# The first attention head's preparation divided anew over the engines, and the low parts of the probabilities dealt out by key tile in another way

## What is computed

```python
def _attn_ref(q, k, v):                      # 2 x 8 heads, 1152 keys, head_dim 64
    q_pool = q.reshape(B, H, S // 2, 2, D).mean(axis=3)      # 576 queries per head
    scores = scale * np.matmul(q_pool, k.transpose(0, 1, 3, 2))
    scores = scores - np.max(scores, axis=-1, keepdims=True)
    attn = np.exp(scores)
    attn = attn / (np.sum(attn, axis=-1, keepdims=True) + 1e-09)
    return np.matmul(attn, v)
def _moe_ref(x, w_in, w_out):                # 1152 tokens, 512 -> 2048 -> 512
    h = x @ w_in
    return (h * np.tanh(softplus(h))) @ w_out
def _moe2_ref(x, w_in, w_out):
    h = x @ w_in
    return np.where(h > 0, h, np.exp(h) - 1) @ w_out
```

## Time and profile before

| | us |
|---|---|
| median of 3 runs | 705.71 |
| lowest and highest | 703.37, 706.11 |
| profiled execution | 703.71 |
| its span | 701.9 |

### The profile page before, as it was taken

One profiled execution on the slowest core, in us unless ns is written; L12 is line 12 of the kernel. 1 busy time (PEld: TensorE's weight loads), 2 busy tenths in 40 slices (PEclk: granted clock), 3 DMA queues, 4 the chain that ended last, 5 costly groups with the idle time before them and its releaser, 6 DMA issues.

```text
span 701.9 us, 12236 instructions
## 1 busy us (share of the span) xinstructions
PE 657.8 (94%) x3984; PEld 636.7 (91%) x3984; DVE 423.4 (60%) x620; ACT 397.0 (57%) x743; POOL 426.5 (61%) x388
## 2 busy tenths in 40 slices
PE   3589999999999999999999999999999999999997
PEld 2478889898898988899999999999999999999997
DVE  6667878787887876377777665777543332223222
ACT  2357888888888878755555555555643322222221
POOL 4266788888888866587786666787644422222221
PEclk9599999999999999999999999999999999999999
DMA  5355564555556540012220000122222110001001
GB/s 162 96 155 157 147 174 135 163 159 158 143 147 163 157 110 16 16 50 71 62 61 0 0 0 30 48 67 67 60 77 61 46 45 0 0 0 46 1 1 45
DMA packets 31503, 54.30 MB, mean 77 GB/s; under 512 B 4752, under 2 KB 10208, under 8 KB 31456
## 3 DMA queue, kind: packets, MB, share of 16 engines
q1 hardware_dynamic: 31296, 53.66, 27.7%
q10 hardware_dynamic: 160, 0.04, 0.0%
HBM read 30.93 MB, written 2.36 MB: 47 GB/s over the span
## 4 chain that ended last, share of the span: by engine, by line
PE 67%; POOL 8%; ACT 8%; DVE 7%; issue 7%; DMA 2%; SPq 1%; POOLq 0%; ACTq 0%; DVEq 0%
PE py L490 9%; PE py L491 8%; PE py L492 8%; PE pH L475 8%; PE pH L476 8%; PE pH L477 8%; PE pm L398 5%; DVE part_max L712 3%; PE po L430 3%; PE po L431 3%; PE po L432 3%; PE ps L413 3%; PE ps L414 3%; POOL pl L931 3%; ACT ph L565 2%
## 5 line engine op out<-in xcount | busy, mean ns | idle before, releaser
L986 POOL TENSOR_TENSOR gl<-fg,gh 128x384 fp32r<-128x384 f32 x96 | 97.3, 1014 | 142.4 <-ACT gh L655 141.1
L931 POOL TENSOR_TENSOR pl<-p,ph 128x576 fp32r<-128x576 f32 x72 | 106.0, 1480 | 67.4 <-ACT p L571 63.3
L712 DVE TENSOR_REDUCE part_max<-pm 128x2 f32<-128x768 f32 (+1 forms) x123 | 111.1, 904 | 39.9 <-PE pm L398 38.1
L490 PE MATMUL py<-gh,wout_h 128*128 128x384 f32 x384 | 129.2, 336 | 3.6 <-DVE xl L842 2.2
L491 PE MATMUL py<-gl,wout_h 128*128 128x384 f32 x384 | 128.4, 334 | 0.0
L492 PE MATMUL py<-gh,wout_l 128*128 128x384 f32 x384 | 128.3, 334 | 0.0
L477 PE MATMUL pH<-xh,win_l 128*128 (+1 forms) x384 | 128.3, 334 | 0.0
L475 PE MATMUL pH<-xh,win_h 128*128 (+1 forms) x384 | 128.3, 334 | 0.0
L476 PE MATMUL pH<-xl,win_h 128*128 (+1 forms) x384 | 128.3, 334 | 0.0
L565 ACT ACTIVATE ph<-ps 128x576 fp32r<-128x576 f32 x144 | 93.9, 652 | 51.2 <-PE ps L414 48.8
L821 DVE RECIPROCAL fi<-fp 128x192 f32<-128x192 f32 x48 | 64.9, 1353 | 52.2 <-POOL fp L994 52.1
(11 more groups left out here) (68 smaller groups left out, 1367.7 us busy)
## 6 DMA issues: line engine op xcount, KB each, us to landing
kh<-k_hi SPq DMA_DIRECT2D x60, 144.0 KB, 2.6
w_raw<-w_in SPq DMA_DIRECT2D x32, 256.0 KB, 2.7
w_raw<-w_out SPq DMA_DIRECT2D x32, 256.0 KB, 2.6
k_pack<-kP SPq DMA_DIRECT2D x16, 288.0 KB, 3.2
q_raw<-qT SPq DMA_DIRECT2D x16, 288.0 KB, 3.1
v_raw<-v SPq DMA_DIRECT2D x16, 288.0 KB, 2.9
kl<-k_pack SPq DMA_DIRECT2D x32, 144.0 KB, 2.4
q<-q SPq DMA_DIRECT2D x16, 144.0 KB, 2.5
```

The costliest lines, as they stand in the source:

```text
L490: pe.matmul(out, hi, gh[:, f % 4, :], start=(f == 0), stop=False)
L712: dve.tensor_reduce(part_max[:, par, 2 * g:2 * g + wide], group_banks(n, g)[:, 0:wide, 0:MC], AX.X, ALU.max).then_inc(m_read, 1)
L931: pool.tensor_tensor(pl[:, ph_slot(slot, kt), :], p32[:, p32_slot(n, kt) % 3, :], ph[:, ph_slot(slot, kt), :].bitcast(F32), ALU.subtract). ...
```

## The change

Start of the program: VectorE sums and rounds head 0's q, and makes both halves of `q1`; keys' upper halves are written by VectorE and the lower ones by ScalarE; the constant row of `kl` is set by ScalarE, the presets of `vt` by GpSimd; SyncE loads q first. Three groups of maxima of head 1 stand ahead of head 0's scores, and ScalarE's preparation of head 2 ahead of the exponentials. Semaphores of presets and of the k loads are doubled, one for each parity.

Steady part: `POOL_KT` gives GpSimd tiles 1, 3, 5, 7 (and 8 in even heads). At tiles 6 and 7 scores and group stand ahead of the value matmuls, as they did at tiles 0 to 5; at tile 8 they still follow. Steps of the division and of the preparation stand at other tiles, and VectorE does the division's steps ahead of `split_p` of the same tile.

```diff
-POOL_KT = ((2, 4, 5, 6, 8), (2, 4, 5, 8))
+POOL_KT = ((1, 3, 5, 7, 8), (1, 3, 5, 7))
-FIRST_GROUPS = (2, 2, 2, 2, 0, 1, 1, 1, 2)
+EARLY_GROUPS = 3
+FIRST_GROUPS = (2, 1, 1, 1, 1, 1, 1, 1, 1)
 GROUPS = (1, 1, 1, 0, 1, 1, 1, 1, 1)
-VECTOR_AT = {"scale": (1, None), "invert_0": (3, None), "invert_1": (5, None), "finalize": (None, 3)}
+VECTOR_AT = {"scale": (0, None), "invert_0": (3, None), "invert_1": (4, None), "finalize": (None, 0)}
...
-GPSIMD_AT = {"split_v": (0, 0), "multiply_sums": (1, None), "sum_q": (3, 3), "split_w": (4, 4),
-             "split_k": (6, 6), "split_q": (7, 7), "split_x": (None, 7)}
+GPSIMD_AT = {"split_v": (1, 1), "multiply_sums": (1, None), "split_w": (3, 3), "sum_q": (3, 3),
+             "split_x": (None, 5), "split_k": (6, 6), "split_q": (8, 8)}
...
                     nxt = ahead(n, kt)
-                    if kt + AHEAD < KT:
+                    if kt == KT - 1:
+                        pv(n, kt)
+                    if nxt is not None:
                         scores(*nxt)
-                        for head, g in groups_at(n, kt):
-                            max_group(head, g)
+                    for head, g in groups_at(n, kt):
+                        max_group(head, g)
+                    if kt < KT - 1:
                         pv(n, kt)
-                    else:
-                        pv(n, kt)
-                        if nxt is not None:
-                            scores(*nxt)
-                        for head, g in groups_at(n, kt):
-                            max_group(head, g)
...
-            preset_scores(0)
+            for par in range(2):
+                dve.memset(kl[par][D:2 * D, :].bitcast(F32), 0.0).then_inc(kl_preset[par], 1)
+                dve.memset(q2[par][D:2 * D, :].bitcast(F32), 0.0).then_inc(q2_preset[par], 1)
+            dve.wait_ge(q_in, 16)
+            dve.tensor_tensor(q_sum[:, :], q_raw[:, 0, :], q_raw[:, 1, :], ALU.add).then_inc(q_summed, 1)
+            dve.wait_ge(q_summed, 1)
+            dve.tensor_copy(q_hi[:, :], q_sum[:, :]).then_inc(first_rounded, 1)
+            dve.wait_ge(first_rounded, 1)
+            for part, cols in ((slice(0, D), slice(0, HQ)), (slice(D, 2 * D), slice(HQ, SQ))):
+                dve.tensor_copy(q1[D:2 * D, 0, cols], q_hi[part, :].bitcast(F32)).then_inc(q1_spread, 16)
+                dve.tensor_tensor(q1[0:D, 0, cols], q_sum[part, :], q_hi[part, :].bitcast(F32),
+                                  ALU.subtract).then_inc(q1_spread, 16)
             dve.wait_ge(k_rounded, 1)
-            for rows in (slice(0, D), slice(D, 2 * D)):
-                for part, cols in ((slice(0, D), slice(0, HK)), (slice(D, 2 * D), slice(HK, SK))):
-                    dve.tensor_copy(kh[0][rows, cols], k_hi[part, :].bitcast(F32)).then_inc(kh_spread, 16)
+            for part, cols in ((slice(0, D), slice(0, HK)), (slice(D, 2 * D), slice(HK, SK))):
+                dve.tensor_copy(kh[0][0:D, cols], k_hi[part, :].bitcast(F32)).then_inc(kh_spread, 16)
```

More of the change, by code:

```diff
@@ L131, in build @@
         w_rd = [sem(f"w_rd{i}") for i in range(2)]
-        preset, preset_kl, preset_pad, preset_vt = sem("preset"), sem("preset_kl"), sem("preset_pad"), sem("preset_vt")
+        preset_pad = sem("preset_pad")
+        q2_preset, kl_preset, vt_preset = [[sem(f"{name}_preset{i}") for i in range(2)] for name in ("q2", "kl", "vt")]
+        first_rounded = sem("first_rounded")
         preset_row, row_reduced, row_spread = sem("preset_row"), sem("row_reduced"), sem("row_spread")
@@ L135, in build @@
         q1_spread, q2_spread = sem("q1_spread"), sem("q2_spread")
-        kl_spread, k_rounded, kp_in = sem("kl_spread"), sem("k_rounded"), sem("kp_in")
+        kl_spread, k_rounded = sem("kl_spread"), sem("k_rounded")
+        kp_in = [sem(f"kp_in{i}") for i in range(2)]
         sum_prod, sum_inv = sem("sum_prod"), sem("sum_inv")
@@ L222, in groups_at @@
             counts = FIRST_GROUPS if n == 0 else GROUPS
[L223 to L227, removed]
+            before = (EARLY_GROUPS if n == 0 else sum(GROUPS[4:])) + sum(counts[:kt])
             for g in range(before, before + counts[kt]):
@@ L337, in next_q @@
                 load_q(m)
+            load_q(0)
             load_kp(0)
-            load_q(0)
             load_kp(1)
@@ L437, in _ @@
                 max_group(0, g)
-            pe.wait_ge(preset, 1)
-            pe.wait_ge(preset_kl, 2)
+            for g in range(EARLY_GROUPS):
+                max_group(1, g)
+            pe.wait_ge(q2_preset[0], 1)
+            pe.wait_ge(kl_preset[0], 2)
             for kt in range(AHEAD):
@@ L538, in split_q, with preset_sign, first_keys @@
                 act.activation(q_hi[:, :], q_sum[:, :], ACT.Copy).then_inc(qh_done, 1)
+            def preset_sign(par):
+                act.wait_ge(kl_preset[par], 1)
+                act.activation(kl[par][D:D + 1, :], kl[par][D:D + 1, :].bitcast(F32), ACT.Copy, bias=-1.0,
+                               scale=0.0).then_inc(kl_preset[par], 1)
+            def first_keys(cols, part):
+                act.wait_ge(k_rounded, 1)
+                act.activation(kh[0][D:2 * D, cols], k_hi[part, :].bitcast(F32), ACT.Copy).then_inc(kh_spread, 16)
             def split_v(n):
@@ L592, in split_x @@
                 act.activation(x_tile(xh, p), x_pair[:, :], ACT.Copy).then_inc(xh_done, 1)
-            split_q(0)
+            preset_sign(0)
             round_k(0)
+            first_keys(slice(0, HK), slice(0, D))
+            first_keys(slice(HK, SK), slice(D, 2 * D))
             split_v(0)
+            round_k(1)
             split_q(1)
-            round_k(1)
+            preset_sign(1)
             spread_row(0)
+            split_q(2)
+            round_k(2)
             for kt in range(AHEAD):
                 exp_tile(0, kt)
-            split_q(2)
-            round_k(2)
             for n in range(HEADS):
@@ L778, in _ @@
                 max_group(0, g)
-            preset_v(0)
-            preset_scores(1)
-            preset_v(1)
+            for g in range(EARLY_GROUPS):
+                max_group(1, g)
             for kt in range(AHEAD):
@@ L790, in _ @@
                         max_group(head, g)
-                    nxt = ahead(n, kt)
-                    if nxt is not None and nxt[1] in VKT[nxt[0] % 2]:
-                        split_p(*nxt)
                     if at("scale"):
@@ L801, in _ @@
                         finalize(n // 2 - 1)
+                    nxt = ahead(n, kt)
+                    if nxt is not None and nxt[1] in VKT[nxt[0] % 2]:
+                        split_p(*nxt)
             scale_by_partner(PAIRS - 1)
@@ L949, in _ @@
             split_k(1)
+            sum_q(2)
+            split_q(2)
             for kt in range(AHEAD):
```

45 lines of the change are left out of this document (17 added, 28 removed).

## The result

The changed kernel takes 708.08 us (median of 12 executions, 705.65 to 709.70), the one before, beside it on the same chip, 703.95 (median of 12). The ratio is 1.005 with an interval of 1.0033 to 1.0066: 0.5% slower, 3.5 us by the ratio and 4.1 by the medians, where the prediction said 8.4. The time lies inside the range of 700 to 720, just under the forecast's own 708.5 to 718. The profiled execution took 706.97, its span is 705.2 for 701.9.

The account below looks back on a forecast made before the run. Attention heads were taken as bound by TensorE's work (14.6 of 16.1 us) plus waits on chains of small operations. Start −6.3 and steady heads +14.7 gave +8.4, hence 712.1 (profiled) or 714.1 (median), forecast 713 us, range 700 to 720.

Parts of the forecast that it names:

- behind tile 2's subtraction: Steady heads: VectorE subtracts tile 2 ahead of reducing tile 0's group, delaying tile 1's group and value matmuls, +0.8 us per head.
- behind the collision: Steady heads, tile 0: scaling or finalizing meets GpSimd's subtraction of tile 3, delaying tile 2's group, +0.6 us per head.
- given back at tile 5 of odd heads: Odd heads: finalizing no longer stands before the reduction of tile 4's group, so tile 5's group waits less, −0.8 us.
- the steady term: Heads 1 to 15 together: odd heads 17.05 for 16.4, even 17.45 for 16.0, +14.7 us, bounds 7 and 19.
- (a): Start: with casts and presets divided anew, the first maximum matmul comes at 9.8 us, 1.9 earlier.
- (b): Start: three groups of head 1 fit into the row of maxima's 3.6 us trip; first scores 22.3, against 24.16.
- (c): Start: the first value matmul still waits for a double group, 30.7 us against 32.5.
- (d): Head 0: seven single groups, 14.6 us of matmuls and about 2 at the low clock; ends at 47.1 against 51.71.
- R1: Rival, faster: steady heads stay at 16.1 us and only the start counts, 699 us; chance 0.17.
- R2: Rival, near no change: wait behind tile 2 but no collision, 0.5 us per head, 707 us; chance 0.15.
- R3: Rival, slower: row of maxima's margin fails, 0.3 us per head more, or start gains 3; 718 us; with R4 0.14.
- R4: Rival: start gets no shorter because q or the GpSimd subtraction comes late, 717 us; chance with R3 0.14.

Follow-up runs that it names:

- e13: Changed kernel, with GpSimd's subtraction of tile 3 waiting, from head 2 on, until VectorE's scaling or finalizing is over: 701.74 us, 0.9963 of the kernel before.
- e6: e4 with the new POOL_KT as the only change in its steady part: 708.78 us, 1.007 of the kernel before.
- e3: Changed kernel with TensorE's old order at tiles 6 and 7, value matmuls ahead of scores and group: 709.13 us, 1.0061 of the kernel before.
- e11: e4 with the loads of the first weights and head 1's v behind the copies of head 2's keys and queries: 693.7 us, 0.9846 of the kernel before.
- e12: e4 with finalizing at the odd head's tile 1, ScalarE's split_x at tile 3, and the loads placed as in e11: 690.27 us, 0.9784 of the kernel before.
- e14: e10 with the loads placed as in e11: 688.84 us, 0.9773 of the kernel before.
- e8: e4 without the three early groups of maxima, head 0 with double groups again: 703.43 us, 0.9999 of the kernel before.
- e10: e4 with finalizing at the odd head's tile 1, ScalarE's split_x at tile 3, and both reciprocals at tile 5: 690.75 us, 0.9801 of the kernel before.
- e1: Changed kernel with only POOL_KT, the tiles GpSimd subtracts, taken back to that of before: 757.31 us, 1.0752 of the kernel before.
- e4: Changed kernel's new start with the whole steady part of before: 696.85 us, 0.9878 of the kernel before.

## Why the prediction was right in direction and more than twice too large

**Right.** A shorter start and longer steady heads, the steady part larger. The two waits per head, by the starts of TensorE's matmuls less their pitch: behind tile 2's subtraction 0.67 (predicted 0.8); behind the collision 0.75 (0.6); 0.77 given back at tile 5 of odd heads (0.8). At the place of the second wait the kernel before lost 0.17 in even heads and 0.07 in odd ones already, so the net is 0.6 to 0.7. `e13` shows the second by taking its cause away, `e6` the first without the second. What the profile was to show is there: x_pair at 1.4 or more, 17 us between copies, waits on the reduction at tiles 1 and 2; first scores near 22.3 and the last copy near 301 are not (24.64 and 297.1). Tiles 6 and 7 cost nothing (`e3`), and the row of maxima stayed hidden in steady heads.

**The step that failed** is the size of the steady term: "Odd: 17.05 for 16.4; even: 17.45 for 16.0" and with it +14.7. Measured: +10.2 for heads 2 to 15 in the profile, where the prediction has 13.8. Of the 3.6 between them 1.5 are in the six even heads (+1.20 each, not +1.45), 0.7 in the five odd ones before head 13 (+0.51, not +0.65), 0.6 in head 13 and 0.85 in heads 14 and 15. The even head's term was also added up loosely: 0.8, 0.6 and 0.2 make 1.6. By the ratios the split is another: the steady part +12.1 ± 1.9 for 14.7 and the start −8.6 ± 1.5 for −6.3. So the steady term was too large by either measure, and how much of the whole miss is the start's stays open between 0.8 and 2.3 us.

In the even heads the walk had the reduction start 0.79 behind the start of VectorE's subtraction. In the trace of before that distance stands where the reduction had to wait for its own input as well; back to back it is 0.61 to 0.68 (175.28 to 175.89, 151.03 to 151.70). The reciprocal's follower also starts 0.97 behind it, not after its whole 1.05. So the group of tile 5 starts 11.64 behind the zero (176.89 less 165.25) instead of the 11.96 of the walk, and an even head gets back 0.25 at tile 5 (and loses 0.1 at tile 7) where the prediction charged 0.2 more. Head 13 was at 16.94 already before the change (+0.07, not +0.65), and heads 14 and 15 lost 0.35 instead of 1.2, which fits that few reductions are left there for the subtraction to stand in front of; it was not tested.

**The start** came out 0.8 better than its sum (−6.24 up to head 1's copy, for −5.4), by steps that were wrong on both sides. (a) 10.22 instead of 9.8: the memsets ended at 5.03 instead of 4.6. The 1.5 that the prediction added for blocked casts was right, though most of it fell elsewhere: the rounding of q took 1.39 for 0.3 to 0.4, and the second key cast 0.93 for 0.46. (b) First scores 24.64 instead of 22.3: the prediction let the row's trip take 3.6 as in the earlier trace rows, but an earlier row meets SyncE's loads, and the trip takes 5.56; `e11`, `e12` and `e14` show their part in it. (c) The first value matmul came at 32.74, 2.0 late by the same delay. (d) Head 0 then needed 14.0 us from its first value matmul to its copy where 16.4 were forecast, for two reasons. The prediction charged a whole head's 14.6 of TensorE work, but scores and groups of tile 0 stand ahead of the first value matmul: what is left is 82 matmuls at 0.133 and seven groups at 0.35, 13.4 us. And the 2 us at the low clock did not come: the value matmuls follow each other at 0.133 from 32.74 on (granted clock 0.70 in 24 to 36, for 0.51 in the earlier trace rows). The worth of the groups without the clock can be read from two runs whose value matmuls are at 0.133 from the first one, `e8` and `e10`: 18.0 and 13.3 us from there to head 0's copy. So single groups for double ones give 4.7 us in head 0 at one and the same clock.

**The base.** 1.8 us of the gap to 713 is no step of the change: the kernel before has a median of 703.95 over 12 executions, against 705.71 over the three of the forecast.

**The rivals.** R1 fell: heads are 1.20 and 0.51 longer. R2 gave the nearest time, 707, for a reason that was wrong: the collision is there in nearly all heads, and what was smaller lay elsewhere. R3 did not come in the changed kernel, but `e1` shows how near it is. R4's early delay was real (0.4 and 2.3 us) and paid back by (d), whose size the prediction had not worked out from the right stretch.

## What to carry to other kernels

Ahead of moving a two-input VectorE operation, look at what GpSimd does in the 1.5 us around the new place; here the move turned 1.13 and 0.84 (0.75 undisturbed) into 1.65 in nearly all heads, and moving it by one tile (or letting GpSimd wait) gave it back in the odd ones. A collision by itself costs nothing, as `e14` shows: it costs where TensorE waits for the reduction behind it. In front of the step that TensorE waits for there must be nothing that could stand behind it: one subtraction in front of one reduction, with the bank that it frees late, cost 0.67 of 16 us, and the best kernel came from keeping the tiles of before, moving two steps of the division and putting two loads behind the row. A time between two rows is a price only if the second row did not wait for its own input.

## What was unexpected of the hardware

- Small casts are held up as well. A cast of 128 x 288 took 1.39 us with GpSimd's subtraction beside it (5.14 to 6.78) and ended 0.16 after it; casts of 64 x 288 took 0.30 undisturbed. In `e4` the subtraction ends 0.09 later and the cast 0.10 later.
- A DMA of 2.5 KB is no small matter when others are under way: 5.56 us from issue to the first matmul behind it at a DMA share of 1.03, 4.04 at 0.99 (`e1`), at most 3.87 at 0.65 (`e11`). In steady heads of the changed kernel, at a share of 0.54, its median from issue to last landing is 1.76.
- TensorE's pace in the start does not repeat. The first value and score matmuls follow each other at 0.24 us (1.2 GHz), later at 0.133 (2.4 GHz). The first pair at the fast pitch starts at 37.3 before, 32.7 after, 36.2 in `e4`, 31.1 in `e8`, 30.6 in `e10`, 37.8 in `e6`. Kernels with the same start (`e4`, `e6`, `e10`) differ by 7 us here, and by 2 us in their first scores (24.82, 24.92, 22.75). A span of one execution can therefore stand some 2 us from the median: `e10`'s span is 1.6 below `e14`'s, though its median is 1.9 above it. That these two account for the scatter of all executions is likely, not shown, since only one of each kernel was traced.
- A granted clock of 1.00 can stand for no record at all. It reads 1.00 in `e11` at 18.5 to 24, where score matmuls (23.43 after 22.95 for two) still follow each other at 0.24: the first clock record of that trace is at 33.4. In the start the distance of matmuls is the surer measure.
